# Expert rows of a mixture-of-experts kernel: fetched as quarters and turned in 32x32 blocks on VectorE

## What is computed

```python
for t in range(S):                       # attention
    state = gamma * state + einsum('bhd,bhe->bhde', k[:, :, t], v[:, :, t])
    y[:, :, t] = scale * einsum('bhd,bhde->bhe', q[:, :, t], state)
logits = x @ w_gate                      # MoE, x is y with heads joined
e_idx = argmax(logits, axis=1)
...
for e in range(E):
    mask = e_idx == e
    h = maximum(x[mask] @ w1[e], 0)
    out[mask] = gate_w * eom * (h @ w2[e])
...
xn = out / rms * rms_g                   # gated MLP
return (silu(xn @ w_gate) * (xn @ w_val)) @ w_out
```

## Time and profile before

| | us |
|---|---|
| median of 3 runs | 1131.57 |
| lowest and highest | 1129.25, 1132.27 |
| the profiled execution | 1131.11 |
| its span in the trace | 1129.3 |
| attention, up to the first expert matmul | 0 to 149.9 |
| MoE tiles 0 and 1 with the routing | 149.9 to 177.1 |
| MoE tiles 2 to 28 | 177.1 to 523.6 |
| MLP | 525.9 to 1129.3 |

### The profile page before, as it was taken

How to read it: one execution, slowest core, us unless ns; L and a number is a source line. 1 busy time by engine, 2 the same in 40 slices (tenths; PEclk the granted TensorE clock), 3 DMA queues, 4 the chain that set the end, 5 groups by cost and what they waited for, 6 DMA issues and landing times.

```text
span 1129.3 us, 20456 instructions
## 1 busy us (share of the span) xinstructions
PE 1106.1 (98%) x6371; PEld 916.4 (81%) x6372; DVE 437.9 (39%) x840; ACT 383.6 (34%) x631; POOL 178.3 (16%) x245
## 2 busy tenths in 40 slices
PE   6999999999999998999999999999999999999998
PEld 5888887888888886887888888888888888888886
DVE  4777757433424325441443322322332242224222
ACT  2445435433525436442223311511331151132112
POOL 2444422322221200010001300110030011001000
PEclk9999999999999999999999999999999999999999
DMA  9998825533344533433201200010020001000001
GB/s 217 236 246 225 237 78 166 176 108 128 112 130 149 186 111 113 132 105 103 75 1 38 75 1 1 38 37 0 0 74 0 0 28 46 0 0 38 1 1 37
DMA packets 111000, 97.39 MB, mean 86 GB/s; under 512 B 80832, under 2 KB 86368, under 8 KB 110944
## 3 DMA queue, kind: packets, MB, share of 16 engines
q1 hardware_dynamic: 95680, 61.88, 20.1%
q0 software_dynamic: 8832, 26.81, 7.1%
q10 hardware_dynamic: 6432, 7.96, 2.2%
HBM read 76.41 MB, written 20.22 MB: 86 GB/s over the span
## 4 chain that ended last, share of the span: by engine, by line
PE 93%; DMA 2%; ACT 2%; DVE 2%; issue 1%; ACTq 1%; POOL 0%; SPq 0%; DVEq 0%; POOLq 0%
PE bank L700 14%; PE bank L702 14%; PE bank L701 14%; PE banks L624 13%; PE bank L597 12%; PE banks L700 3%; PE banks L702 3%; PE banks L701 3%; PE bank L507 2%; PE banks L493 2%; PE bank L537 2%; PE bank L545 1%; PE bank L466 1%; PE banks L612 1%; PE bank L612 1%
## 5 line engine op out<-in xcount | busy, mean ns | idle before, releaser
L1345 DVE TENSOR_TENSOR gated<-bank,sig 128x512 f32<-128x512 f32 x72 | 49.8, 692 | 353.8 <-ACT sig L976 353.8
L976 ACT ACTIVATE sig<-bank 128x512 f32<-128x512 f32 x72 | 43.1, 598 | 327.3 <-PE bank L702 317.1
L700 PE MATMUL bank<-xh,w1h 128*128 128x512 f32 x384 | 149.4, 389 | 0.0
L701 PE MATMUL bank<-xl,w1h 128*128 128x512 f32 x384 | 149.4, 389 | 0.0
L702 PE MATMUL bank<-xh,w1l 128*128 128x512 f32 x384 | 149.4, 389 | 0.0
L701 PEld LDWEIGHTS bank<-xl,w1h 128*128 128x128 f32 x384 | 72.1, 188 | 15.0
L700 PEld LDWEIGHTS bank<-xh,w1h 128*128 128x128 f32 x384 | 72.1, 188 | 14.9
L702 PEld LDWEIGHTS bank<-xh,w1l 128*128 128x128 f32 x384 | 72.1, 188 | 14.9
L983 ACT ACTIVATE hh<-prod 128x512 fp32r<-128x512 f32 x72 | 45.5, 632 | 110.7 <-DVE prod L1349 110.7
L1354 DVE TENSOR_TENSOR hl<-prod,hh 128x512 fp32r<-128x512 f32 x72 | 49.9, 693 | 54.1 <-ACT hh L983 54.1
L1542 POOL DMA_INDIRECT out_rows<-x_out,cur_idx x10 | 10.1, 1007 | 382.3 <-ACT x_out L990 291.4
(11 more groups left out here) (240 smaller groups left out, 2163.0 us busy)
## 6 DMA issues: line engine op xcount, KB each, us to landing
stage<-in_moe_w SPq DMA_DIRECT2D x64, 512.0 KB
expert_rows<-tile_o ACTq DMA_DIRECT2D x29, 256.0 KB
q_raw<-in_q SPq DMA_DIRECT2D x24, 256.0 KB
k_raw<-in_k SPq DMA_DIRECT2D x24, 256.0 KB
v_raw<-in_v SPq DMA_DIRECT2D x24, 256.0 KB
stage<-in_moe_w_out SPq DMA_DIRECT2D x6, 512.0 KB
stage<-in_moe_w_gate SPq DMA_DIRECT2D x5, 512.0 KB
stage<-in_moe_w_val SPq DMA_DIRECT2D x5, 512.0 KB
```

Source lines behind the costliest of these rows:

```text
L700: pe.matmul(out_ap, lh, rh, start=first, stop=False)
L701: pe.matmul(out_ap, lh, rl, start=False, stop=False)
L976: nc.scalar.activation(sig[:], bank[GV[f % 2][0]][:, :], ACT.Sigmoid).then_inc(s["sig_done"], 1)
L1345: v3.tensor_tensor(gated[:], bank[GV[f % 2][0]][:, :], sig[:], ALU.mult).then_inc(s["gated_done"], 1)
```

## The change

The DRAM table `x_rows` is addressed as quarters: row r, quarter q is row 4r + q of a table of 128 elements. A fetch of a tile is now four indirect DMAs of 128 quarter rows each (512 bytes), one for each column block `part` of `xg`; partition p gets quarter p // 32 of row 32 * part + p % 32. DVE turns `xg` in place with one instruction over 128 x 512, which transposes each block of 32x32 (`STREAM_TRANSPOSE`). Read through the view `turned_rows`, that is the transposed tile, with the features in another order over the partitions; the rows of `w1` are loaded in that same order, by four groups of 32 partitions. ACT's `rows_hi` and DVE's `rows_lo` read `xg` in SBUF and no longer the bank. PE's `turn_rows` is gone. The next fetch waits on `tileT_lo` (both parts made) and no longer on `tile_turned`. The index table has four entries to a tile, which costs DVE one more instruction in the routing and wider ones; the constants for it move from `con` to `con_a`, which grows by 227 columns while `con` loses 118.

```diff
@@ SP
+            w1_rows = w1.rearrange("e (q b j) f -> b e q j f", q=QUARTERS, j=BLOCK)
...
@@ PE
-            def turn_rows(a):
-
-                pe.wait_ge(s["rows_in"], 16 * (a + 1))
-                if not (isinstance(a, int) and a < 1):
-                    pe.wait_ge(s["tileT_lo"], a)
-                for i in range(KD):
-                    mm = pe.transpose(quad(XG_T)[:, i, :], xg[:, i * P:(i + 1) * P], ident)
-                mm.then_inc(s["tile_turned"], 1)
...
                 for g in range(2):
-                    if g and not (isinstance(a, int) and a == TILES - 1):
-                        turn_rows(a + 1)
                     pe.wait_ge(s["relu_done"], 2 * a + g + 1)
...
-            pe.wait_ge(s["state_ready"], with_state(last))
-            turn_rows(0)
             outputs(last)
...
@@ ACT
-                nc.scalar.activation(xgh[:], quad(XG_T), ACT.Copy).then_inc(s["tileT_hi"], 1)
+                nc.scalar.activation(xgh[:], turned_rows, ACT.Copy).then_inc(s["tileT_hi"], 1)
...
@@ DVE
+            def turn_rows(a):
+                dve.wait_ge(s["rows_in"], 16 * QUARTERS * (a + 1))
+                v3.transpose(xg[:], xg[:]).then_inc(s["tile_turned"], 1)
 
             def turned_lo_parts(a):
                 for g in range(2):
+                    if g == 0 and not (isinstance(a, int) and a == TILES - 1):
+                        turn_rows(a + 1)
                     if g and not (isinstance(a, int) and a == TILES - 1):
                         rows_lo(a + 1)
                     dve.wait_ge(s["hTh"], 2 * a + g + 1)
...
@@ POOL
+                for part in range(QUARTERS):
+                    at = a * QUARTERS + part
+                    nc.gpsimd.indirect_dma_start(xg[:, part * P:(part + 1) * P].bitcast(U32), None, x_quarters,
+                                                 bass.IndirectOffsetOnAxis(lead_idx[:, at:at + 1], 0))\
+                      .then_inc(s["rows_in"], 16)
...
             for a in range(1, LEAD):
-                pool.wait_ge(s["tile_turned"], a)
+                pool.wait_ge(s["tileT_lo"], a)
                 fetch_lead(a)
...
-                pool.wait_ge(s["rows_in"], 16 * a)
-                nc.gpsimd.tensor_copy(cur_idx[:], row_idx[:, ds(a, 1)]).then_inc(s["idx_staged"], 1)
+                pool.wait_ge(s["rows_in"], 16 * QUARTERS * a)
+                nc.gpsimd.tensor_copy(cur_idx[:], row_idx[:, ds(a, 1), :]).then_inc(s["idx_staged"], 1)
                 pool.wait_ge(s["idx_staged"], a - LEAD + 1)
-                pool.wait_ge(s["tile_turned"], a)
+                pool.wait_ge(s["tileT_lo"], a)
```

More of the change, by code:

```diff
@@ L28 @@
 LEAD_UNITS = 20
+QUARTERS = 4
+BLOCK = 32
 TILES = (TOKENS - EXPERTS) // P + EXPERTS + LEAD
@@ L94, in constants @@
     a[:, A_STRICT:A_STRICT + P] = p < j
+    a[:, A_TILE:A_TILE + UNITS] = P * np.arange(UNITS)
+    a[:, A_NUM:A_NUM + TILES + 1] = np.arange(TILES + 1) - LEAD
+    a[:, A_TID:A_TID + UNITS] = P * np.arange(UNITS)[None, :] + p
+    quarter = p // BLOCK
+    rows = BLOCK * np.arange(QUARTERS)[None, None, :] + (p % BLOCK)[:, :, None]
+    for at, tiles in ((A_ROW, np.arange(TILES + 1) - LEAD), (A_LEAD, np.arange(LEAD))):
+        numbers = QUARTERS * (P * tiles[None, :, None] + rows) + quarter[:, :, None]
+        a[:, at:at + numbers[0].size] = numbers.reshape(P, -1)
+    a[:, A_QTR:A_QTR + 1] = quarter
     return c.astype(np.float32)
@@ L1446, in fetch_rows @@
                 pool.sem_inc(s["stood"], 1)
-                nc.gpsimd.indirect_dma_start(xg[:].bitcast(U32), None, x_dram, bass.IndirectOffsetOnAxis(cur_idx[:, 0:1], 0))\
-                  .then_inc(s["rows_in"], 16)
+                for part in range(QUARTERS):
+                    nc.gpsimd.indirect_dma_start(xg[:, part * P:(part + 1) * P].bitcast(U32), None, x_quarters,
+                                                 bass.IndirectOffsetOnAxis(cur_idx[:, part:part + 1], 0))\
+                      .then_inc(s["rows_in"], 16)
             early = [(g01h, g01l), (v01h, v01l)]
```

78 lines of the change are left out of this document (45 added, 33 removed).

## The result

| | before | after |
|---|---|---|
| median, us | 1131.92 (1129.25 to 1133.96, 4 runs) | 1173.0 (1167.85 to 1176.96, 4 runs) |
| the profiled execution | 1131.11 | 1167.85 |
| its span | 1129.3 | 1166.1 |
| first expert matmul | 149.87 | 166.48 |
| start of tile 2 | 177.11 | 197.11 |

The changed kernel is slower by the ratio 1.0371 (95% interval 1.0344 to 1.0398), 41 us. The forecast was 1135.0, the range ended at 1142.0. In the profiled executions 16.6 us are lost before PE starts the experts and 22.6 between the first and the last tile; some 2 come back behind that. (The profiled execution of after is the fastest of its four.)

What follows compares the result with a forecast made beforehand. PE, busy for 98% of the span, was taken as the bound, its transposes hidden behind ACT. Removed 0, steady tiles 0, moved 0 and the start's +3.4 on the median 1131.57 gave 1135.0; range 1131.6 to 1142.

Steps and rivals of the forecast that it cites:

- Moved: the rows of `w1`: Weight loads: w1 in another row order has the same 4 KB rows, so it costs 0.
- Added on POOL: three more DMAs to a fetch: Every fetch: 1.25 us each on POOL, last quarter issued 3.75 after the first; cost in steady tiles 0.
- 4.6 us to spare: Steady tiles: rows need 7.1 us of the 11.7 between xgl and the time they must be in xg.
- rival 4: Rows come late in the tiles, POOL's DMAs stretched beside DVE's work: 1140 for some, 1149 for a quarter of tiles; 12%.
- the start: First expert tiles: tile 0 +1.5, tile 1 +3.3 in all, tile 2 +0.1 us.
- Removed: the transposes: PE between the hidden groups: 12.6 us leave its queue, 0 on the path, since they fill a hole ACT makes.
- Rival 1: PE's transposes were on the path, so 12.6 us come free and the time is 1122.4; 7%.
- Added on DVE: 0.7: The block transpose of 128x512 takes 0.7 us, range 0.6 to 1.36; cost in steady tiles 0.
- Tile 0: First expert tile: PE waits for the last quarter, its turn and the split, +1.5 us (1.0 to 3.0).
- Tile 1: Second expert tile: rows land last, just; PE's wait grows to some 2.3 us, +3.3 in all (+2.0 to +6.6).
- rival 3: PE's clock falls behind the longer pauses at the start, 1.3 us a fall: 1136.3 for one, 1137.6 for two; 18%.

Runs made afterwards that it cites:

- stored_order: The changed kernel with w1 loaded in whole blocks, the column order made where the attention stores x: 1148.85 us.
- before_extra_lead: The kernel before with three more small indirect DMAs behind tile 0's lead fetch, into a buffer nobody reads: 1137.1 us.
- scatters_apart: stored_order with the two scatters of each of tiles 6 to 15 issued ahead of the fetch, not right behind its four DMAs: 1146.89 us.
- first_fetch_whole: scatters_apart with tile 0 fetched by one indirect DMA of whole rows: 1142.72 us.
- one_fetch: stored_order with one indirect DMA of 2 KB rows for each fetch in place of four: 1133.77 us.
- one_fetch_late: one_fetch with the fetch of the next tile held back until PE is through with the current one: 1142.48 us.
- before_one_turn: The kernel before with one of PE's four row transposes in every tile but the first: 1133.17 us, ratio 1.0013.
- before_groups_4: The kernel before with nothing changed but w1 loaded by four groups of 32 rows: 1173.03 us.
- before_groups_8: The kernel before with w1 loaded in 8 groups of 16 rows: 1145.49 us.
- own_buffer: stored_order with DVE's turn written to PSUM bank XG_T, so the next fetch waits for the turn alone: 1166.06 us.
- before_extra_fetches: The kernel before with three more indirect DMAs behind the fetch of 14 tiles (4 to 17), into unused SBUF: 1135.79 us.

## Why the prediction was wrong

**Moved: the rows of `w1`, "the same 4 KB rows. Both 0."** This is the step that failed. The rows are the same and the bytes are the same; what changed is the slowest dimension of the pattern, from 128 to 4, and with it the DMA engines at work, from 16 to 4. Alone it costs 42.0 us. Neither the sum nor a rival had it; the term was closed by looking at the size of the rows, and no row that the prediction used has the DMA share of a stretch with a weight load alone (the earlier trace rows is the fetch of rows, 0.68 and 222 GB/s). The next term, at 0 in steady tiles, failed as well, and would by itself have broken the range: stored_order, with whole loads, is at 1148.85, past 1142.

**Added on POOL: three more DMAs to a fetch.** Their price on POOL was right: issued at 157.87, 159.15, 160.40 and 161.66 in after, 1.25 to 1.28 apart, and DVE turns at 164.33, 2.67 behind the last (2.5 predicted). What they do to others was not, in two places. "Both are done before PE starts the experts" holds (in after the scatter ends at 164.02 and PE starts at 166.48), but it looks only at what is queued on POOL, and not at engines with nothing to do with POOL: before_extra_lead measures 5.9 us for the three DMAs alone. And 4.6 us to spare in a steady tile was worked out with a landing of 2.5; under weight loads it took up to 7.0. This is rival 4, for which the prediction had 12% and 1140 to 1149. Its place was right (rows late in some tiles) and so was stored_order's size, 1148.85, but the releaser was the landing and POOL's own weight split; of POOL's DMAs stretched, as the rival had it, little is seen: those of a fetch take 1.035 us (mean) in after where before has 0.989.

**The 17.8 us that are left with whole loads** come apart as differences of medians: 4.2 for the lead fetch in four (scatters_apart less first_fetch_whole), 2.0 for scatters right behind a fetch (stored_order less scatters_apart), 8.9 for four DMAs to a fetch in the other tiles (first_fetch_whole less one_fetch; 8.7 was measured for lateness alone in one_fetch_late, so held-up signals need not be in it), and 2.7 for the rest (one_fetch less before). Some 3.4 of the first and 3.3 of the 8.7 are estimated to be clock. The last is near what the sum had under the start less the DMAs. The intervals are about 2 us wide on each kernel, and the kernels ran on several chips, so 2.0 and 2.7 are known in sign and size only roughly.

**Removed: the transposes, 0.** Right, shown by before_one_turn for three of the four. Rival 1 fell. (28 of them stand in the gaps, not 29: turn_rows(0) does not; 12.0 us and not 12.6.)

**Added on DVE: 0.7.** Right: 697 to 714 ns. Steady tiles without a weight load take 12.49 in after as in before, as predicted.

**Tile 0: +1.5.** With one DMA it is +0.95 (150.82 in one_fetch); the 3.75 of three more DMAs didn't add their own length but 5.0 in stored_order (155.80). In after it is +16.6, and 14.9 of that is there before the fetch is issued (157.87 for 142.95), which is the grouped loads' part (before_groups_4 has +20.4 in all). From the fetch to the first expert matmul it is 8.61 in place of 6.92, +1.7 for +1.5 predicted.

**Tile 1.** The turn does stand behind the routing. Timeline of after:

```profile
190.16 0.36 DVE L1250 TENSOR_TENSOR z<-bank,top 128x192 f32<-128x192 f32 x1 [0.49 <-DVE whole L1246]
...
190.44 0.70 DVE L1133 STREAM_TRANSPOSE xg<-xg 128x512 f32<-128x512 f32 x1
191.06 0.65 DVE L1143 TENSOR_TENSOR hidl<-bank,hidh 128x512 fp32r<-128x512 f32 x1
...
191.77 1.92 PE L628 MATMUL banks<-w2h,hidl 128*128 128x512 f32 x4 [2.34 <-DVE hidl L1143]
```

PE waits 2.34 there, where the earlier trace rows has 0.46; the prediction had "some 2.3". It named the landing as last, just; the two come together: `z` ends at 190.52 and the turn starts with it, and the landing is there by 190.38, when POOL, which waits for it too, goes on. Tile 0's and tile 1's parts are 3.6 us in all, for 3.3 predicted: the sum of the start was right, behind loads that made it late. Behind the wait the clock falls:

```profile
192.00:196.00 4.00, 4.00 (x12) 3.09 (x12) 3.83 (x8) 4.00 (x7) 2.09 (x3) 0.58 0.24 86
```

PEclk 0.58 is near the lower of TensorE's two levels, 1.2 GHz, behind a pause of 2.34; 12 matmuls ran in 4 us (20 do in 242 to 246 of before_groups_8, above). Tile 1 takes 16.65 in after and 13.30 in before; less some 1.9 for the longer wait, some 1.4 is the clock, near the 1.3 that rival 3 (18%) named for one fall.

**The clock as a whole.** Rival 3 was true at more places than this one. After is granted the lower level (0.50) at 52.0, 127.1, 192.0, 434.3 and 475.3 for 3.4 us each and at 219.3 for 10.2; before at 527.2 alone, for 3.4. PE works some 20 us in these stretches of after and 3.4 in that of before; taken as half as fast there, an estimated 8 of the 36.7 us between the profiled executions are clock. stored_order has 20.0 us of PE's work in such stretches, also an estimated 8 more than before. The falls shown here (192, 219.3) stand behind or in pauses that the late rows and weights make, so the clock is no cause of its own; but it is inside the costs above, and rivals 3 and 4 could come true together. Ahead of the MLP it went the other way: before pauses 2.28 and then falls to 0.51, after pauses 1.8 there and doesn't fall, and its MLP is 1.8 us shorter.

**The range.** It was built from what could be bounded by rows of before. The cost that broke it was held at nothing without a row, and had no upper end at all; the spare time of the steady tiles was worked out with a landing of 2.5, and the rival that had it later stood mostly outside the range.

## What to carry to other kernels

When an edit changes the pattern of a load, compare the DMA share and the GB/s of a stretch that has only that load, before any talk of bytes or row sizes: with the outermost dimension at 4 the same 512 KB came at 98 GB/s in place of 396, and everything behind it on the queue came late too. A DMA split into several isn't paid on its issuing engine alone: ask what the row of issues pushes back, and what it does to the signals of engines that have nothing to do with it. A term set to nothing needs a row that shows the nothing.

## What the runs showed of the hardware

- **SP is held while it issues a load over few DMA engines, and what stands behind it on the queue.** Of four such pieces of 512 KB in a row the first three take 0.55 to 0.67 us to be issued and the fourth 2.50 (203.32 in after; 2.16 to 3.59 over the six such places), where a piece in whole blocks never takes more than 0.38 (48 in before). The attention's loads of `v_raw` behind them take 2.40 us (median, at most 5.27) for 0.37 (at most 1.00), one of `k_raw` 5.96. The pieces land one behind another, the third some 22 us after its issue.
- **Five or six indirect DMAs in a row on GpSimd hold up signals between other engines** in some places: in the three timelines above the waiting engine starts 3.3, 6.6 and 3.3 us behind the end of what it needs (xT and `pick` in before_extra_lead; `hid` in own_buffer, where ACT is busy for 1.4 of it; `tile_o` in before_extra_fetches). Between 190 and 430 such waits sum to 52.4 us in 7 of `tile_o` in before_extra_fetches and 19.4 in 7 of `hid` and 21.2 in 3 of `tile_o` in own_buffer; before has none. Rows of four do it rarely: one_fetch has a single such wait of 0.7, behind a row of four, and scatters_apart one of `tile_o` of 7.0 (530.31, 2.1 past PE's end), also behind a row of four. What it is that is held isn't settled: the record has PE's matmuls done, and the ACT and DVE waits shown above end within 1.3 us of the last issue. In before_extra_lead PE's own matmuls are held too. Nor is it a rule without exception: before has a row of eight in the MLP (926.7 to 936.7) and no such wait there, and after has a row of six in ten tiles and one of five at the lead fetch, and no such wait between 20 and 165 or between 190 and 560. What sets after apart from stored_order there, which has 15.5 us of `hid` in 6 waits and 8.3 of `tile_o` in one, stays open.
- **A 32x32-block transpose of 128 x 512 float32 on VectorE takes 0.70 us** (697 to 714 ns), in place in SBUF, and 0.72 (714 to 728 ns) from SBUF into a PSUM bank (own_buffer).
